# Attention as a chunked recurrence: scores from one 64x128 stationary part, the state of two heads in one product, and the outputs of a tile in one PSUM bank

## What is computed

```python
# r, k, v: batch 4, heads 8, sequence 768, head size 48, fp32; w, u: 8 x 48
for t in range(S):
    cur = einsum('bhd,bhe->bhde', u * k_t, v_t)
    y_t = einsum('bhd,bhde->bhe', r_t, state + cur)
    state = w[..., None] * state + einsum('bhd,bhe->bhde', k_t, v_t)
x = y.transpose(0, 2, 1, 3).reshape(3072, 384)
# then: x @ w_gate (384 x 8) ranks the tokens, each of 8 experts takes 384 of them,
# h = relu(x @ w1[e]) @ w2[e];  out = ((h @ w_a) * (h @ w_b)) @ w_out
```

## Time and profile before

| | |
|---|---|
| median of 3 runs | 904.5 us (902.1 to 906.38) |
| the profiled execution: its time, its span | 903.44 us, 901.5 us |
| TensorE busy with matmuls | 831.6 us, 92% of the span |
| VectorE, ScalarE, GpSimd busy | 538.3, 234.6, 425.8 us |
| mean granted clock of TensorE | 0.964 |
| attention, first matmul to last logits | 7.47 to 155.96 us |
| routing of the first expert, with the clock at half | 156 to 202 us |
| experts and bilinear layer | 202 us to the end |

### The profile page before, as it was taken

How to read it: one execution, slowest core, us unless ns; L and a number is a source line. 1 busy time by engine, 2 the same in 40 slices (tenths; PEclk the granted TensorE clock), 3 DMA queues, 4 the chain that set the end, 5 groups by cost and what they waited for, 6 DMA issues and landing times.

```text
span 901.5 us, 19288 instructions
## 1 busy us (share of the span) xinstructions
PE 831.6 (92%) x7941; PEld 798.6 (89%) x7941; DVE 538.3 (60%) x1294; ACT 234.6 (26%) x494; POOL 425.8 (47%) x448
## 2 busy tenths in 40 slices
PE   5898987329999999999999999999999999999994
PEld 5798887219999999999999999999999999999994
DVE  6675765657776676677657675777576422631221
ACT  2233322021223123312322232223222222331221
POOL 5666764067047605751673177217622770475001
PEclk9999999559999999999999999999999999999998
DMA  9997951031012102210121122012101220121000
GB/s 171 204 226 169 223 134 47 1 113 55 1 59 80 55 1 71 77 46 14 66 79 37 36 65 67 27 36 80 54 27 36 88 59 12 60 82 53 1 1 27
DMA packets 94023, 61.82 MB, mean 69 GB/s; under 512 B 79344, under 2 KB 83952, under 8 KB 93936
## 3 DMA queue, kind: packets, MB, share of 16 engines
q0 software_dynamic: 11008, 34.61, 12.5%
q1 hardware_dynamic: 78640, 21.25, 11.9%
q10 hardware_dynamic: 4288, 4.72, 1.5%
HBM read 51.13 MB, written 9.44 MB: 67 GB/s over the span
## 4 chain that ended last, share of the span: by engine, by line
PE 76%; DVE 3%; issue 1%; DMA 1%; POOL 1%; ACT 0%; ACTq 0%; POOLq 0%; DVEq 0%
PE bank L1252 41%; PE bank L1326 17%; PE bank L1295 11%; PE bank L1308 2%; PE bank L1275 2%; PE bank L1312 1%; DVE mask_mem L682 1%; PE bank L1192 1%; DMA wst<-in_moe_w,rows_i 1%; PE bank L1243 1%; PE bank L1208 1%; PE bank L1200 1%; PE bank L1233 0%; POOL w L502 0%; DVE cand L678 0%
## 5 line engine op out<-in xcount | busy, mean ns | idle before, releaser
L1252 PE MATMUL bank<-act,w_all 128*128 128x384 f32 x1584 | 295.9, 338 | 0.0
L1252 PEld LDWEIGHTS bank<-act,w_all 128*128 128x128 f32 x1584 | 275.3, 188 | 0.0
L485 POOL DMA_INDIRECT wst<-in_moe_w,rows_i x48 | 52.3, 1090 | 246.3 <-DVE rows_i L752 190.9
L1326 PE MATMUL bank<-w_all,gs 128*128 128x384 f32 x864 | 167.4, 337 | 0.3 <-DVE gs L875 0.3
L502 POOL TENSOR_TENSOR w<-wst,w 128x384 fp32r<-128x384 f32 (+1 forms) x106 | 130.6, 1232 | 43.9 <-ACT w L1016 38.2
L1326 PEld LDWEIGHTS bank<-w_all,gs 128*128 128x128 f32 x864 | 150.0, 188 | 0.6 <-DVE gs L875 0.6
L1295 PE MATMUL bank<-hs,w 128*128 128x384 f32 x576 | 113.1, 340 | 0.0
L872 DVE TENSOR_TENSOR ga<-ga,bank 128x384 f32<-128x384 f32 x96 | 53.0, 552 | 86.2 <-PE bank L1252 80.6
L1295 PEld LDWEIGHTS bank<-hs,w 128*128 128x128 f32 x576 | 100.6, 188 | 0.0
L1037 ACT ACTIVATE gs<-ga 128x384 fp32r<-128x384 f32 x96 | 50.5, 526 | 187.2 <-DVE ga L872 187.2
L1252 PE MATMUL bank<-act,w 128*128 128x384 f32 x504 | 98.5, 339 | 0.0
(11 more groups left out here) (179 smaller groups left out, 1047.0 us busy)
## 6 DMA issues: line engine op xcount, KB each, us to landing
kt<-in_k SPq DMA_DIRECT2D x24, 192.0 KB, 4.1
rt<-in_r SPq DMA_DIRECT2D x24, 192.0 KB, 4.7
vt<-in_v SPq DMA_DIRECT2D x24, 192.0 KB, 4.9
x_rows<-xs ACTq DMA_DIRECT2D x24, 192.0 KB, 3.4
raw<-in_moe_w_a SPq DMA_DIRECT2D x6, 384.0 KB, 4.8
raw<-in_moe_w_b SPq DMA_DIRECT2D x6, 384.0 KB, 5.3
raw<-in_moe_w_out SPq DMA_DIRECT2D x6, 384.0 KB, 5.2
wst<-in_moe_w,rows_i POOLq DMA_INDIRECT x112
```

The lines of the kernel that those rows point to most:

```text
L485: pool.indirect_dma_start(wst[:, k % STAGES, :], None, w1_rows, bass.IndirectOffsetOnAxis(ap=rows_i[:, k:k + 1], axis=0)).then_inc(wst_lan ...
L1252: last = pe.matmul(dst, wt(a), mv(b), start=(n == 0 and (a, b) == (0, 0)), stop=(n == len(pairs) - 1 and (a, b) == (1, 0)))
L1326: last = pe.matmul(acc[t][:, 0:D], gs2[:, c % 2, a, t * P:t * P + P], wo2[:, b, c, :], start=(c == 0 and (a, b) == (0, 0)), stop=(c == FFC ...
```

## The change

The score product of a head takes all 128 keys as one stationary part of 64x128 (8 products a tile instead of 16). The state of a pair is kept as one 128x96 block: the even head's state in rows 0 to 63 and columns 0 to 47, the odd one's in rows 64 to 127 and columns 48 to 95, with zeros between, which come from `w128`: its cross entries are zero, so that `fade` makes them zero in each tile. `from_state` then takes both heads of a pair in one product with 128 rows and 96 moving columns (8 products instead of 16). All outputs of a tile lie in one bank, and the tiles take banks 5 and 6 in turn, so `outputs` is one operation over 128x384 instead of two over 128x192, and the waits for it are one tile later. `total`, `state`, `fade` and `add_update` become twice as wide. `ktab` gets its room in `rk`.

```diff
@@ -136,9 +136,8 @@
             causal = at("causal", [P, P])
             decay = at("decay", [P, PAIRS, HALF + 1])
             decay_rev = at("decay_rev", [P, PAIRS, HALF + 1])
-            w128 = at("w128", [P, PAIRS, 1])
+            w128 = at("w128", [P, PAIRS, 2])
             rtab = at("rtab", [P, PAIRS, P])
-            ktab = at("ktab", [P, PAIRS, P])
             ktab_tok = at("ktab_tok", [P, PAIRS, P])
             u_col = at("u_col", [P, PAIRS, 1])
             uw = at("uw", [P, PAIRS * H])
@@ -149,11 +148,12 @@
             rs = at("rs", [P, 3, PAIRS, P])
             ks = at("ks", [P, 2, PAIRS, P])
             rk = at("rk", [P, 2, PAIRS, P])
+            ktab = rk[:, 1, :, :]
             am = at("am", [P, 2, 2, PAIRS, P])
             dsum = at("dsum", [P, 2, H])
             dv = at("dv", [P, 2, H, DH])
-            total = at("total", [P, PAIRS, DH])
-            state = at("state", [P, 2, PAIRS, DH])
+            total = at("total", [P, PAIRS, 2 * DH])
+            state = at("state", [P, 2, PAIRS, 2 * DH])
             xs = at("xs", [P, 2, D])
             xt = at("xt", [P, DC, P])
             raw = at("raw", [P, RAWS, PIECE])
@@ -256,8 +256,7 @@
         pA = [bank[2][:, :].rearrange("p (h t) -> p h t", t=P), bank[3][:, :].rearrange("p (h t) -> p h t", t=P)]
         pU = bank[4][:, 0:PAIRS * DH].rearrange("p (a e) -> p a e", a=PAIRS)
         pD = bank[7][:, D + E:D + E + H]
-        pY = [bank[5][:, 0:PAIRS * DH].rearrange("p (a e) -> p a e", a=PAIRS),
-              bank[6][:, 0:PAIRS * DH].rearrange("p (a e) -> p a e", a=PAIRS)]
+        pY = [bank[5][:, 0:D], bank[6][:, 0:D]]
         pXT = bank[7][:, 0:D].rearrange("p (c t) -> p c t", c=DC)
         pL = bank[7][:, D:D + E]
         acc = [bank[n] for n in range(3)]
@@ -386,6 +385,7 @@
             step(pool.affine_select(out=ident[:, :], in_=ident[:, :], compare_op=ALU.not_equal, fill=1.0,
                                     base=0, pattern=[[-1, P]], channel_multiplier=1))
             assert made[0] == CP_IDENT + 1
+            pool.memset(w128[:, :, :], 0.0)
             step(pool.memset(uw[:, :], 0.0))
             step(pool.memset(ktok[:, :, :, DH:HALF], 0.0))
             step_wait(pool.memset(causal[:, :], 1.0))
@@ -447,7 +447,9 @@
                 pool.wait_ge(total_ready, updates(n))
                 if n >= 2:
                     pool.wait_ge(y_done, n - 1)
-                pool.tensor_tensor(state[:, n % 2, :, :], total[:, :, :], w128[:, :, :].to_broadcast([P, PAIRS, DH]),
+                pool.tensor_tensor(state[:, n % 2, :, :].rearrange("p a (h d) -> p (a h) d", h=2),
+                                   total[:, :, :].rearrange("p a (h d) -> p (a h) d", h=2),
+                                   w128[:, :, :].rearrange("p a (h o) -> p (a h) o", o=1).to_broadcast([P, H, DH]),
                                    ALU.mult).then_inc(state_ready, 1)
 
             def lower_raw(n):
@@ -571,8 +573,12 @@
                 step(dve.tensor_tensor(rtab[:, :, HALF - 2 * n:HALF - n], rtab[:, :, HALF - n:HALF],
                                        rtab[:, :, HALF - n:HALF - n + 1].to_broadcast([P, PAIRS, n]), ALU.mult))
                 n *= 2
-            step(dve.tensor_tensor(w128[:, :, :], decay[:, :, HALF:HALF + 1], decay[:, :, HALF:HALF + 1], ALU.mult))
             dve.wait_ge(s_cpool, CP_IDENT + 2)
+            for h2 in range(2):
+                rows = HALVES[h2]
+                last = dve.tensor_tensor(w128[rows, :, h2:h2 + 1], decay[rows, :, HALF:HALF + 1],
+                                         decay[rows, :, HALF:HALF + 1], ALU.mult)
+            step(last)
             dve.wait_ge(s_u, 32)
             for h2 in range(2):
                 rows = HALVES[h2]
@@ -614,21 +620,21 @@
                 if n >= 2:
                     dve.wait_ge(x_stored[n % 2], 16 * (n // 2))
                     dve.wait_ge(x_turned, n - 1)
-                xs4 = xs[:, n % 2, :].rearrange("p (a h d) -> p a h d", a=PAIRS, h=2)
-                dv4 = dv[:, n % 2, :, :].rearrange("p (a h) d -> p a h d", h=2)
-                for h2 in range(2):
-                    last = dve.tensor_tensor(xs4[:, :, h2, :], pY[h2], dv4[:, :, h2, :], ALU.add)
-                last.then_inc(x_ready, 1)
+                dve.tensor_tensor(xs[:, n % 2, :], pY[n % 2], dv[:, n % 2, :, :].rearrange("p h d -> p (h d)"),
+                                  ALU.add).then_inc(x_ready, 1)
 
             def add_update(n):
 
                 dve.wait_ge(update_done, updates(n + 1))
                 if n:
                     dve.wait_ge(state_ready, n // TPB * STATES + n % TPB)
+                both = pU.rearrange("p a (o d) -> p a o d", o=1).to_broadcast([P, PAIRS, 2, DH])
+                total4 = total[:, :, :].rearrange("p a (h d) -> p a h d", h=2)
                 if n % TPB:
-                    ins = dve.tensor_tensor(total[:, :, :], state[:, n % 2, :, :], pU, ALU.add)
+                    ins = dve.tensor_tensor(total4, state[:, n % 2, :, :].rearrange("p a (h d) -> p a h d", h=2), both,
+                                            ALU.add)
                 else:
-                    ins = dve.tensor_copy(total[:, :, :], pU)
+                    ins = dve.tensor_copy(total4, both)
                 ins.then_inc(total_ready, 1)
 
             scale_r(0)
@@ -1084,30 +1090,31 @@
                     pe.wait_ge(am_ready, 2 * n)
                 for a in range(PAIRS):
                     for h2 in range(2):
-                        for jh in HALVES:
-                            last = pe.matmul(pA[h2][jh, a, :], ks[HALVES[h2], n % 2, a, jh],
-                                             rs[HALVES[h2], n % 3, a, :], start=True, stop=True)
+                        last = pe.matmul(pA[h2][:, a, :], ks[HALVES[h2], n % 2, a, :],
+                                         rs[HALVES[h2], n % 3, a, :], start=True, stop=True)
                 last.then_inc(a_done, 1)
 
             def from_state(n):
 
                 pe.wait_ge(state_ready, n // TPB * STATES + n % TPB)
-                pe.wait_ge(x_ready, n)
+                if n >= 2:
+                    pe.wait_ge(x_ready, n - 1)
                 for a in range(PAIRS):
-                    for h2 in range(2):
-                        for ih in HALVES:
-                            pe.matmul(pY[h2][ih, a, :], rs[HALVES[h2], n % 3, a, ih], state[HALVES[h2], n % 2, a, :],
-                                      start=(a == 0), stop=False, skip_group_check=True)
+                    for ih in HALVES:
+                        pe.matmul(pY[n % 2][ih, a * 2 * DH:(a + 1) * 2 * DH], rs[:, n % 3, a, ih],
+                                  state[:, n % 2, a, :], start=(a == 0), stop=False, skip_group_check=True)
 
             def values(n):
-                if n >= 1:
-                    pe.wait_ge(x_ready, n)
+                if n >= 2:
+                    pe.wait_ge(x_ready, n - 1)
                 for h2 in range(2):
                     pe.wait_ge(am_ready, 2 * n + h2 + 1)
                     for a in range(PAIRS):
+                        o = (2 * a + h2) * DH
                         for ih in HALVES:
-                            last = pe.matmul(pY[h2][ih, a, :], am[:, n % 2, h2, a, ih], vt[:, n % SLOTS, 2 * a + h2, :],
-                                             start=(n % TPB == 0 and a == 0), stop=(a == PAIRS - 1),
+                            last = pe.matmul(pY[n % 2][ih, o:o + DH], am[:, n % 2, h2, a, ih],
+                                             vt[:, n % SLOTS, 2 * a + h2, :],
+                                             start=(n % TPB == 0 and a + h2 == 0), stop=(a + h2 == PAIRS),
                                              skip_group_check=True)
                 last.then_inc(y_done, 1)
```

## The result

The changed kernel takes 891.42 us (median of 4 runs, 890.64 to 892.73) against 904.56 us (902.1 to 906.38): a ratio of 0.986, 95% interval 0.983 to 0.988, 13 us faster. The forecast was 895 us, in a range of 887 to 907. The profiled execution took 890.64 us, span 888.7.

The account below looks back on a forecast made before the run. TensorE bounds attention, with 11.6 us of stalls on late instruction packets. Stalls -9.7, clock -4.2, shape change +3.8, slips +0.5, start +0.2 sum to -9.4 us: 903.4 becomes 894.0, with 1.1 for the median 895 us, range 887 to 907.

Parts of the forecast that it names:

- Stalls: TensorE's waits for late instruction packets in attention: 11.6 us before, 1.9 left with fewer instructions, so 9.7 us saved.
- Clock: Granted clock in attention: no fall after the three long stalls any more, 3 x 1.4 = 4.2 us saved, bounds 0 and 5.1.
- Scores: Score product of a tile, 16 instruction pairs instead of 32 at twice the pitch: 0.82 us, no gain; upper bound 1.7.
- State product: Product with the state in a tile, 16 pairs at 39 ns: 0.63 us against 0.66; upper bound 1.25.
- `fade`: GpSimd's operation ahead of the state product: from 531 to 831 ns, 0.3 us to spare, so nothing on the path.
- `xs` and `total`: VectorE in attention: `total` from 342 to some 552 ns, `outputs` from 2 x 348 to 552; the two cancel.
- Start: Start of the kernel: `w128` made by two operations instead of one, the first `ktok` waits for them, +0.2 us.
- the last logits: Sign at the end of attention: its last logits come at 147 us.
- The tile: Sign on TensorE: the tile at the end of attention takes 5.3 us, where an undisturbed one took 5.15.
- the distance from scores to values: Sign within a tile on TensorE: 1.67 us instead of 1.48, 0.19 us for each of 20 tiles, +3.8 us.
- the number of packets: Sign on the instruction queue: about 20 instruction packets where there were 25.
- the term of +0.5 us for slips of these engines: Allowance for slips in GpSimd and VectorE from the wider operations in attention, +0.5 us.

Follow-up runs that it names:

- the kernel without transfers: The kernel before with neither the reloads of k, r and v after the sixth tile nor the later weight pieces; 889.25 us.
- the slowed kernel: The kernel before with one more, unused 128x128 by 512-column fp32 product in each tile from the third; 912.2 us.
- without the reloads: The kernel before, loading k, r and v for the first six tiles only and working on these again later; 896.5 us.
- without the pieces: The kernel before, loading only the first three of 18 pieces of later weights during attention, k, r and v as before; 900.81 us.
- the run with a quarter left out: The changed kernel with scores in four 64x64 parts and, from the second tile, the masked quarter of the scores left out; 899.09 us.
- in the changed kernel, with or without transfers: The changed kernel, and the same without the reloads of k, r and v and the later weight pieces; 892.09 us without them.
- with the scores alone: The kernel before with only the score product's stationary part made 64x128, outputs still in two banks, waits as before; 892.98 us.
- the state's half: The changed kernel with the scores back in four 64x64 parts, keeping paired state, one output bank per tile and later waits; 897.93 us.
- the kernel with wide values: The kernel before with the product of masked scores and values as one 128x128 stationary part, 8 products instead of 16; 911.88 us.

## Why the prediction was right

The mechanism was the one forecast: with fewer instructions in a tile a packet has more time. The places of the stalls show that they are late packets, the kernel without transfers that traffic makes them late, and the slowed kernel that time alone takes stalls away. Step by step:

- Stalls: forecast 9.7 of 11.6 us saved, 1.9 left. 10.8 went, and 0.8 is left. The forecast left 0.7 us to each of three long stalls because it took the time between two packets there for fixed at 6.6 us. From one place with remainder 194 to the next TensorE took 6.7 to 6.9 us at these in before, 6.1 to 6.6 without the reloads, 5.6 to 6.6 without the pieces, 5.2 and 5.3 without both. In the changed kernel it took 6.9 us once, with the 0.8 us of stall, and nowhere else over 6.2 between 20 and 130 us. So of the three stalls of 0.7 us that the forecast left one came, and two did not. The packets start sooner there (1.4 us on average after the place before, instead of 2.1); why, no run tells. The forecast also left out the 7 instructions of a tile that only wait: it is 309 and 245, not 302 and 238, which makes a packet last 4.3 and 5.7 us and changes little.
- Clock: forecast 4.2 us, and there is indeed no window below the full clock between 20 and 128 us. Attention of before is 13.9 us longer than without transfers, of which the stalls are 8.8 (11.6 and 2.8 us). The other 5.0 us are the three falls of the clock and whatever else the transfers cost; the forecast's bound was 5.1.
- Scores: forecast 0.82 plus the gap, 1.03; 1.10 came. The term was sized by streamed columns. In the run with a quarter left out 64x64 parts did not go by these; for the 64x128 part no run varies the columns.
- State product: forecast 0.63, measured 0.63, two 128x64 parts side by side with 96 columns. Scores and state product together: +0.25 us from scores to values instead of +0.19.
- `fade`: forecast to end 0.3 us ahead of its reader; it ends 0.37 ahead. `xs` and `total` as forecast. Start: the first score load at 13.55 us instead of 13.38, +0.17 for a forecast of 0.2.
- Against the sentences that the prediction weighed. The Trainium skill, "Runtime: NRT & Kernel Launch", section "Instruction fetch mechanics", calls the fetch of instructions hidden. Here it is not, as the 47 stalls at equal counts show. The Trainium skill, "TensorE: Matmul & The Clock Gate", Part 3, section "The mechanism", lets a weight load overlap only with a matmul in flight of another group of rows. By that the state product with 128 rows would have taken 1.7 us; it took 0.63, so loads do overlap there with a matmul of the same rows. The Trainium skill, "TensorEngine Tiling (Array Packing)", section "Key Properties", says that a change of tiling mode drains TensorE. TensorE's loads now stand still for 0.13 us between scores and state product (123.20 to 123.33 us), where before they followed without a gap. That agrees, but from 64x64 to 128x64 parts the loads of before stood still for only 0.05 us, so the price is not one number.

The sum of terms as one tile and the forecast price them is -11.6 - 4.2 + 20 x 0.27 + 0.2 = -10.2 us, and attention became 13.4 us shorter. The traces without transfers show where most of the rest is. A single undisturbed tile went from 5.15 to 5.42 us, but not every tile of before takes 5.15: in its trace without transfers, complete tiles take 5.15 to 5.5 us. A batch of six tiles takes 30.9 us there (a stall left out) and 31.4 in the changed kernel, with or without transfers: +0.5 us and not 5 x 0.27 = 1.35, some 2 us for the four batches. With 10.8 for the stalls and 5.0 for the clock the sum is -10.8 - 5.0 + 2 + 0.2 = -13.6 us. The forecast of 895 was 3.6 us too high because each of the three large terms came out 0.8 to 1.8 us better than forecast. Of its signs, the last logits missed the most: 147 us was forecast, 142.4 measured. The tile (5.3 and 5.42 us), the distance from scores to values (1.67 and 1.73 us) and the number of packets (20 and 21) came as forecast; of the 2 to 4 us of stalls 0.8 came.

Why tiles of before differ in length I read from traces only. In the kernel before without transfers the 5.41 us come where `xs` is late out of VectorE, and there `rk` seems to wait for GpSimd: 1303 ns each before, 871 now. With the wider `fade`, `rk` comes while `fade` runs and goes on right behind it, at 122.96 in the rows above, and GpSimd's `ktok` is the one that takes longer (1.46 us there, 1.01 in the earlier trace rows). What this is worth is not shown: with the scores alone `rk` still takes 1288 ns, and a batch takes 31.4 us as well. So the term of +0.5 us for slips of these engines stays open.

Of the 13.4 us, 0.6 was given back between the end of attention and the end of the span. The runs differ by up to 3 us there, so this says nothing of the change.

## What to carry to other kernels

An engine that issues many small instructions also consumes its program, here 16 KB for each 256 instructions in 4.4 us, and these bytes share the DMA engines with the data. If such an engine idles with nothing to wait for, count its instructions up to each idle time: here all of them stood a multiple of 256 apart. See also whether the idle times go where traffic is thin. A list of waits can put such a stall down to an engine that had long been done, or whose result isn't needed yet. Then fewer and larger instructions pay even if the array works longer on them, as here 5.42 us for 5.15; what they cost depends on the shape, so price the weight load of a wider part by itself.

## What the runs showed of the hardware

- Small fp32 products go by the shape of their stationary part: a 128x128 part with 48 moving columns goes at 120 ns a pair, 128x64 parts side by side at 29 ns, 64x128 parts side by side at 1.10/16 = 69 ns with the gap behind them, and 64x64 parts at 26 ns, which 25% fewer columns did not shorten.
- TensorE's program comes in packets of 16384 bytes, one for 256 instructions, which took 0.9 to 2.3 us each between 20 and 125 us. When one started late, TensorE stood still and went on 1.2 to 1.7 us after it had landed, in 48 stalls of eleven runs.
- Either of two kinds of transfer alone keeps long stalls (5.2 and 4.6 us for the three, 6.3 with both kinds there); with both gone, 1.2 us for two are left. Leaving out one kind saves 1.1 or 1.7 us of them, leaving out both 5.1.
- A stall of 2 us was followed by a fall of the clock in the kernel before, three times of three; one of 1.76 us in the slowed kernel wasn't, without the reloads a fall came after 1.9 us and none after 1.5 and 1.8, without the pieces none after 1.9 and one after 1.7; in the state's half falls came after stalls of 0.9 and 1.5 us, and in the kernel with wide values once with no stall over 0.35 us before it. The length of one stall doesn't decide it.
- An empty semaphore increment on TensorE takes about 0.1 us: 128 of them ahead of the program moved the first matmul by 13.1 us.
